# Spreading the first MLP block's statistics over eight rounds and moving one small addition from VectorE to GpSimd

## The reference, cut to what matters

```python
q_rot, k_rot = rotate(q), rotate(k)                      # rotary tables
scores = q_rot @ k_rot.T / sqrt(64)                      # 576 x 576 a head
attn = exp(scores - max)                                 # row maximum
attn = attn / (sum(attn) + 1e-9)                         # the epsilon the change moves
x = attn @ v                                             # (4, 576, 512) over the heads
xn = (x - mean(x)) / sqrt(var(x) + 1e-6) * g_ln          # first MLP block
x = x + relu(xn @ w_ch1) @ w_ch2
...                                                      # second MLP block, gated
```

## Time and profile before

| what | us |
|---|---|
| three runs | 930.75, 930.87, 931.57; median 930.87 |
| the profiled execution | 931.98 |
| its span (first to last recorded instruction) | 930.2 |
| start of PE's round 2 and of its round 15, from the span's start | 46.64 and 277.94 |
| busy: PE, PEld, DVE, ACT, POOL | 905.6, 840.1, 705.7, 543.7, 551.0 |

### The profile page before, as it was taken

The page is one execution under the profiler, slowest core; times in us unless marked ns, Lnnn a source line. Parts: engine busy times, 40 slices in busy tenths (PEclk is TensorE's granted clock), DMA queues, the critical chain, the costliest instruction groups (busy, mean ns, idle before and its releaser), DMA issues.

```text
span 930.2 us, 18233 instructions
## 1 busy us (share of the span) xinstructions
PE 905.6 (97%) x6153; PEld 840.1 (90%) x6153; DVE 705.7 (76%) x1155; ACT 543.7 (58%) x1184; POOL 551.0 (59%) x547
## 2 busy tenths in 40 slices
PE   4999999999999999999999999999999999999998
PEld 3899999999989999999899988899988989989897
DVE  4799899999998899942777878789998672663623
ACT  3899999999889666543655655565565221212110
POOL 4989899999883477665566668758986210010100
PEclk9999999999999999999999999999999999999999
DMA  6233333334314233100000000002200001010011
GB/s 181 68 98 94 83 93 96 82 93 97 84 43 113 70 96 120 35 1 1 1 1 1 1 1 1 1 2 68 90 26 1 1 1 46 1 50 8 1 47 57
DMA packets 49737, 45.51 MB, mean 49 GB/s; under 512 B 18880, under 2 KB 39616, under 8 KB 49536
## 3 DMA queue, kind: packets, MB, share of 16 engines
q1 hardware_dynamic: 49232, 44.26, 17.4%
q10 hardware_dynamic: 432, 0.30, 0.1%
HBM read 28.81 MB, written 4.72 MB: 36 GB/s over the span
## 4 chain that ended last, share of the span: by engine, by line
PE 85%; DVE 9%; ACT 2%; issue 2%; DMA 1%; SPq 1%; ACTq 0%; DVEq 0%
PE fc_ps L2145 16%; PE seven_ps L2175 14%; PE ring_ps L2041 8%; PE wide_ps L2344 6%; PE scores_ps L1977 6%; PE bank_ps L2300 5%; PE wide_ps L2323 5%; PE bank_ps L2358 5%; PE ring_ps L1988 5%; PE seven_ps L2225 2%; DVE lefts L1651 2%; PE seven_ps L2145 2%; DVE hid_sums L1639 2%; PE scores_ps L1970 2%; PE ring_ps L1923 2%
## 5 line engine op out<-in xcount | busy, mean ns | idle before, releaser
L2145 PE MATMUL fc_ps<-xT,W1s 128*128 128x512 f32 (+1 forms) x828 | 191.0, 380 | 0.4 <-ACT hid L1159 0.3
L2175 PE MATMUL seven_ps<-rights,lefts 128*128 128x256 f32 x1344 | 173.6, 284 | 0.0
L2175 PEld LDWEIGHTS seven_ps<-rights,lefts 128*128 128x128 f32 x1344 | 169.5, 191 | 4.4
L2145 PEld LDWEIGHTS fc_ps<-xT,W1s 128*128 128x128 f32 x828 | 146.2, 189 | 27.7 <-ACT hid L1159 1.3
L1465 DVE TENSOR_REDUCE nmax<-scores_ps 128x1 f32<-128x576 f32 x144 | 106.4, 749 | 17.8 <-PE scores_ps L1977 11.7
L958 POOL TENSOR_TENSOR rights<-w_rest,rights 128x256 fp32r<-128x256 f32 x84 | 80.9, 963 | 54.6 <-ACT rights L1202 54.6
L1065 ACT ACTIVATE E<-scores_ps,nmax 128x576 f32<-128x576 f32 x128 | 95.4, 747 | 10.7 <-DVE nmax L1465 9.9
L1474 DVE TENSOR_TENSOR prob_lo<-ring_ps,prob_hi 128x512 fp32r<-128x512 f32 x144 | 95.3, 681 | 2.4 <-ACT prob_hi L1079 1.9
L1020 POOL TENSOR_TENSOR rstd<-ve,power 128x1 f32<-128x1 f32 x18 | 14.5, 807 | 138.7 <-DVE ve L1833 138.7
L1977 PE MATMUL scores_ps<-stack 128*128 128x288 f32 x384 | 90.0, 321 | 1.2 <-DMA swapped_k<-stack 0.8
L1079 ACT ACTIVATE prob_hi<-ring_ps 128x512 fp32r<-128x512 f32 x144 | 85.3, 610 | 6.4 <-PE ring_ps L1988 5.7
(11 more groups left out here) (185 smaller groups left out, 2066.0 us busy)
## 6 DMA issues: line engine op xcount, KB each, us to landing
swapped_k<-stack SPq DMA_DIRECT2D x32, 144.0 KB, 2.5
stack<-stack SPq DMA_DIRECT2D x32, 144.0 KB, 2.4
w_raw<-in_w SPq DMA_DIRECT2D x18, 256.0 KB, 3.0
qk_raw<-in_k SPq DMA_DIRECT2D x16, 256.0 KB, 2.8
v_raw<-in_v SPq DMA_DIRECT2D x16, 256.0 KB, 2.8
qk_raw<-in_q SPq DMA_DIRECT2D x15, 256.0 KB, 2.8
w_rest<-in_w SPq DMA_DIRECT2D x7, 512.0 KB, 4.5
out<-out_sb SPq DMA_DIRECT2D x14, 256.0 KB, 2.3
```

The lines of the kernel that those rows point to most:

```text
L2145: mm = nc.tensor.matmul(fc1_bank(n, f)[:, 0:cols], W1s[:, slot1(f), w, c, :], xT[:, x, c, 0:cols], start=first, stop=(c == DC - 1 and x == 1))
L2175: mm = nc.tensor.matmul(seven_ps[k][:, 2 * P * a:2 * P * (a + 1)], lefts[:, k, x, P * a:P * (a + 1)], rights[:, k, w, :], start=(g == 0 an ...
```

## The change

Four things. `LOOP` ends at 8 instead of 12: rounds 4 to 7 run in the hardware loop, rounds 8 to 17 are written out on every engine. The statistics of tile t of the first block are taken in round 8 + t; `mean_variance` follows in round 11 and `inverse_std` a round later on GpSimd. Tiles 0 and 1 are normalised in round 13, tile 2 in round 14, tile 3 in round 15. And `denominators` goes from DVE (behind `maximum(r, 4)`) to GpSimd, behind `v_low(r - 1)` and ahead of the products `cross`; there it adds a tile of 1e-9 (`least`, in the memory of what was a gap) and waits for the same nine exponentials of pair r-1, for `rinv_kept` and for the last `write_y` that read its buffer. `reciprocals` stays on DVE.

```diff
-        sbuf(att, "gap", [P, 384])
+        least = sbuf(att, "least", [P, 384])
...
-        LOOP = (4, 12)
+        LOOP = (4, 8)
...
+            nc.gpsimd.memset(least[:, 0:NQK], 1e-9).then_inc(zeroed, 1)
...
+            def denominators(p):
+
+                if not live(p):
+                    return
+                pool.wait_ge(expd, last_of(exp_order, p, range(NQK)))
+                at_least(pool, rinv_kept_s, p - 2, p.i - 1)
+                wait_freed(pool, p - 2, "OA", 0)
+                nc.gpsimd.tensor_tensor(rinv[:, p.odd, 0:NQK], rowsum[:, p.odd, :], least[:, 0:NQK], ALU.add).then_inc(sums_ready, 1)
+
             def keep_rinv(p):
...
-                if is_round(p, PAIRS - 4):
+                if is_round(p, PAIRS - 5):
                     inverse_std(0)
...
             def body(r):
                 scale(r + 1, 1)
                 v_low(r - 1)
+                denominators(r - 1)
                 first_weights(r)
                 crosses(r + 1, 1, 1)
...
-            def denominators(p):
-
-                if not live(p):
-                    return
-                dve.wait_ge(expd, last_of(exp_order, p, range(NQK)))
-                at_least(dve, rinv_kept_s, p - 2, p.i - 1)
-                nc.vector.tensor_scalar(rinv[:, p.odd, 0:NQK], rowsum[:, p.odd, :], 1e-9, None, ALU.add).then_inc(sums_ready, 1)
...
                 maximum(r, 4)
-                denominators(r - 1)
                 reciprocals(r - 1)
...
-                if is_round(r, PAIRS - 4):
+                if is_round(r, PAIRS - 5):
                     mean_variance(0)
...
-                if is_round(r, PAIRS - 4):
+                if is_round(r, PAIRS - 8 + t):
                     tile_statistics(0, t)
-                if is_round(r, PAIRS - 2):
+                if is_round(r, PAIRS - 3 + t // 2 + t // 3):
                     normalise(0, (t,))
```

More of the change, by code:

```diff
@@ L892, in inverse_std @@
                 nc.gpsimd.tensor_tensor(rstd1[:, 0:nt], ve1[:, 0:nt], power[:, 0:nt], ALU.pow).then_inc(rstd_s, 1)
-            pool.wait_ge(zeroed, 2)
+            pool.wait_ge(zeroed, 3)
             def first_w1(f):
```

## The result

The changed kernel takes 946.94 us (median of four runs, 945.22 to 947.93) against 930.81 us for the kernel before on the same chip: ratio 1.0170, interval 1.0158 to 1.0182. The forecast was 946.2 us, in a range of 938 to 957. The profiled execution took 947.15 us with a span of 945.4, so 15.17 us more than the one of before.

What follows compares the result with a forecast made beforehand. PE bounded the kernel before, at 17.36 us a round; GpSimd's circle would bound rounds 2 to 14. Its 15.15 us plus 0.2 for the last tile, added to 930.87, gave 946.2 us, range 938 to 957.

Steps and rivals of the forecast that it cites:

- The addition's wait: On GpSimd behind `v_low`, the addition waits 5.09 us for ACT's ninth exponential, delaying the rotary instructions queued behind it.
- 3.75 of room: How much later, in us, GpSimd's products may start before PE waits for their low parts in its next round.
- The circle: Rounds 2 to 14: PE's L1938, ninth exponential, GpSimd's addition, low parts, next L1938; 18.95 us a round against PE's 17.36.
- The addition itself: Duration of the 128 x 9 addition on GpSimd, taken as 0.18 us, with ends of 0.1 and 0.81.
- Which rounds: Round 1 loses 0.1 us, thirteen rounds, 2 to 14, take 18.95 each; round 15 starts at 293.09, 15.15 us later.
- The 4.78 us of DVE's late rounds: Excess of rounds 12 to 14 over 17.36 us each, ascribed to DVE; already contained in the 15.15 us loss.
- PE idle about 1.6 us a round: Expected sign: PE idle ahead of L1923 and L1938, released by GpSimd's `qk_low`, about 1.6 us a round.
- The last tile in round 15: Its normalisation on DVE falls outside the rounds GpSimd bounds: between 0 and 0.7 us, taken as 0.2.
- the sum of 15.35 us: Forecast growth of the span: 15.15 us up to round 15 plus 0.2 for the last tile.
- Rival A: GpSimd's wait is covered and DVE was the bound in rounds 12 to 14: 4.78 us back, 926.1 us; chance 0.08.
- Rival B: PE's pauses drop TensorE's clock to 1.2 GHz, doubling the circle's 5.75 us first part: 75 us more, 1021 us; chance 0.04.
- Rival C: Loss and win cancel in the same circle, with rounds of 17.73 us instead of 18.95: 930.9 us; chance 0.03.

Runs made afterwards that it cites:

- E2: The kernel before with only the epsilon addition moved from VectorE to GpSimd, behind `v_low`: 948.15 us, ratio 1.0176.
- E3: The changed kernel with GpSimd's addition moved five products later, ahead of `qk_high`: 930.54 us, 0.9991 of the kernel before.
- E5: The changed kernel with one extra GpSimd product, read by nothing, directly behind the addition in rounds 1 to 14: 960.66 us, ratio 1.0314 to the kernel before.
- E12: E5 with a longer extra GpSimd instruction, a power of 128 x 4 for the product: 969.73 us, 1.0411 of the kernel before.
- E11: E3 with rounds 8 to 11 of SyncE, ScalarE and TensorE put back into the hardware loop: 932.00 us, 0.9999 of the kernel before.
- E4: The kernel before with only its loop's end changed from 12 to 8: 932.42 us, ratio 1.0008.
- E10: E3 with only SyncE's rounds 8 to 11 put back into the hardware loop: 930.96 us, 0.9989 of the kernel before.

## Why the prediction was right

- **The addition's wait, 5.09 us in the first round with the old timing, against 3.75 of room.** Right: E2 loses 16 to 17 us with it alone, E3 nothing, with the place moved to where the wait is covered. The decision whether the change loses was made by this one subtraction.
- **The circle, 18.95 us.** Measured 18.94 over thirteen rounds. Its parts in round 9: 5.77 to the end of the exponential (5.75 forecast), 0.08 of hand-over (0.1), 0.16 from the addition's start to the next (0.18), 12.71 for the eleven others (12.82), 0.11 to PE (0.1); 18.83 in that round. The durations of the earlier trace rows held under the new timing.
- **The addition itself.** I took 0.18 between 0.1 and 0.81; its row has 0.21, and 0.16 to the next start.
- **Which rounds.** Thirteen rounds, as forecast. Round 1 did not lose its 0.1 us: PE waits 0.82 us at the start of round 2, but the pause of 1.32 us is gone, and the round is 18.14 long against 18.15 before. Round 15 starts at 292.45 instead of the forecast 293.09; this execution had come to round 2 earlier, at 46.22 against 46.74.
- **The 4.78 us of DVE's late rounds vanish inside the circle.** Right but for some 0.6 us: rounds 12 to 14 take 18.85, 19.19 and 19.01 us, rounds 8 to 11 18.81 to 18.84. PE has still one wait for DVE in them (0.77 us ahead of L1990 at 262.73).
- **PE idle about 1.6 us a round.** The size is right, the sign was too simple: PE's rows show 0.65 to 0.91 us ahead of L1940 and, in six rounds, 0.25 to 0.48 ahead of L1925. In round 9 PE is busy for 17.95 of 18.83 us (the row below), where before it was for 17.35 of 17.35. Of the 1.48 us more, 0.88 are idle and 0.60 are busy time, in which PE does the same work. So the idle time on PE's rows is here less than what the wait costs.

```profile
178.91:197.74 18.83, 17.95 (x145) 17.26 (x145) 15.74 (x27) 16.98 (x39) 15.98 (x16) 1.00 0.33 85
```

- **The last tile in round 15, 0.2 us.** Mis-sized: behind round 15's start the span is 945.4 - 292.45 = 652.95 us, before 930.2 - 277.94 = 652.26, so 0.69 more. That the sum of 15.35 us comes so near the 15.17 of the profiled execution is in part luck: 0.64 too much up to round 15 and 0.49 too little behind it nearly cancel. The longest idle time there that the kernel before does not have is not a wait for VectorE but a pause of PE's score tile 4, which no term of the sum held:

```profile
304.66 0.37 PE L1972 MATMUL scores_ps<-stack 128*128 128x288 f32 x1 [0.59 <-issue]
```

- **Rival A, 926.1 us.** Its condition is met in E3 and its price does not come: 930.54 us. The step that fails is "that is what the change can win". I counted every microsecond above 17.36 in rounds 12 to 14 as DVE being late through these instructions, though PE's waits for `prob_lo` come to 2.2 us and, with 1.02 us for `sum_o` in round 14, its recorded waits for VectorE in these rounds to 3.1; and I priced the same instructions in rounds 8 to 11 at nothing.
- **Rival B, 1021 us.** Rightly unlikely for this change, but not for the reason given, and priced wrongly. In E5 and E12 the clock fell in three and four of these rounds, behind pauses as short as 0.61 and 0.83 us, and kept in others behind longer ones; a single pause in the earlier trace rows that kept its clock was weak evidence. And a fall costs such a round 1.5 to 1.8 us, not 5.75, since the lower clock lasted some 3.4 us there and not the whole first part.
- **Rival C, 930.9 us.** The circle is not shorter than its rows.

## What to carry to other kernels

Before an instruction with a wait is put into an in-order queue, subtract the time at which that queue reaches it from the time at which its producer is done, and compare the difference with the slack of whatever stands behind it: a 0.21 us addition cost 16 us here because eleven instructions for the next round stood behind it, and nothing five products later. If the late engine feeds the engine that feeds the wait, the loss is not paid once but becomes a circle, and its length, added up along its instructions, is the new round. What an engine's excess over the shortest round comes to is not yet what moving its work can win: price the work in the place where it goes as well.

## What the runs showed of the hardware

**Two small VectorE instructions end with an instruction of GpSimd.** `mean_variance`'s addition of 128 x 4 took 1.54 us in the kernel before, 1.70 in E11, 0.76 in E4 and 0.32 in the changed kernel. Each with GpSimd's rows beside it, first the kernel before:

```profile
242.26 1.54 DVE L1528 TENSOR_TENSOR ve<-mv,ve 128x4 f32<-128x4 f32 x1
```

```profile
241.57 1.46 POOL L830 TENSOR_TENSOR rot<-qk_raw,rotary 128x576 f32<-128x576 f32 x1
242.98 0.80 POOL L845 TENSOR_TENSOR cross<-qk_raw,rotary 128x288 f32<-128x288 f32 x1
```

E11:

```profile
226.57 1.70 DVE L1531 TENSOR_TENSOR ve<-mv,ve 128x4 f32<-128x4 f32 x1
```

```profile
227.39 0.86 POOL L846 TENSOR_TENSOR cross<-qk_raw,rotary 128x288 f32<-128x288 f32 x1
```

E4:

```profile
243.98 0.76 DVE L1528 TENSOR_TENSOR ve<-mv,ve 128x4 f32<-128x4 f32 x1
```

```profile
243.26 1.46 POOL L830 TENSOR_TENSOR rot<-qk_raw,rotary 128x576 f32<-128x576 f32 x1
244.66 0.82 POOL L845 TENSOR_TENSOR cross<-qk_raw,rotary 128x288 f32<-128x288 f32 x1
```

And the changed kernel, in round 12:

```profile
238.09 0.32 DVE L1531 TENSOR_TENSOR ve<-mv,ve 128x4 f32<-128x4 f32 x1
```

```profile
236.81 1.59 POOL L877 TENSOR_TENSOR v_split<-v_raw,v_split 128x640 fp32r<-128x640 f32 x1
```

They end at 243.80, 228.27, 244.74 and 238.41; an instruction of GpSimd ends at 243.78, 228.25, 244.72 and 238.40. So the addition's own work is short, and the rest is GpSimd's: in the kernel before and in E11 over two of its instructions (in E11 L831 ran ahead of the row shown, from 226.01 to 227.50), in E4 only up to the end of the first, though GpSimd went straight on with the next. Which of the two happens is open. The row sum's addition on VectorE, 165.11 + 1.00 = 166.11, ends the same way, 0.03 us behind GpSimd's work (166.51 - 0.43 = 166.08). PE pays for it: in E11 it waits 1.28 us for the `prob_lo` behind. The Trainium skill's page "SBUF — State Buffer" (Who interferes with whom) says that a VectorE instruction with two inputs in SBUF contends with a GpSimd instruction that reads SBUF, and that the port pair the two share is an exclusive lock; the rows of `mean_variance`'s addition, which has two such inputs, agree, and add that GpSimd's next instruction can keep it blocked.

**Long DMA issues beside instruction packets.** In E4's written-out rounds some issues of SyncE took 1 us longer. The issue of the K swap's tail in E4, the packet of the same 2 us, and PE's score tile 4, which by the program waits for this swap (its row names no releaser); then the same issue in the kernel before:

```profile
195.20 2.33 SPq L738 DMA_DIRECT2D stack<-stack  x2
```

```profile
q8 instruction: 1, 0.02, 3.8%
```

```profile
198.82 0.37 PE L1970 MATMUL scores_ps<-stack 128*128 128x288 f32 x1 [0.56 <-issue]
```

```profile
194.98 1.24 SPq L738 DMA_DIRECT2D stack<-stack  x2
```

E4's rounds 10 and 11, with a pause of 0.56 and 0.48 us ahead of score tile 4, took 18.13 and 18.04 us against 17.40 and 17.34 before, which is most of the 1.76 us that E4's rounds 8 to 11 lose. With SyncE's own rounds in the loop (E10) issues of 2.10 and 2.15 us still stand beside packets at 194 and 210 us; with ScalarE's and TensorE's in the loop too (E11) there is neither in rounds 8 to 11, though VectorE and GpSimd are still written out. So the packets go with ScalarE's or TensorE's code and not with SyncE's. That they cause the long issues was not shown by itself, and not every packet has a long issue beside it.
